# One reciprocal over 512 suffix products in place of the second scan of each attention chunk

## What is computed

```
state = zeros(B, H, D, D)
for t in range(S):
    state = alpha[:, :, t, :, None] * state + einsum('bhd,bhe->bhde', k[:, :, t], v[:, :, t])
    y[:, :, t] = einsum('bhd,bhde->bhe', q[:, :, t], state)
...
h = relu(xt @ w_tok1) @ w_tok2;  u = x + h.T
h2 = relu(u @ w_ch1) @ w_ch2;    x = u + h2
... then one expert (w1, w2) for each token, picked by a sticky gate
```

## Time and profile before

| | us |
|---|---|
| median of 3 runs | 518.74 (516.93 to 519.31) |
| profiled execution, its own time | 517.57 |
| its span, first to last instruction | 515.8 |
| PE busy in it | 455.6 (88%) |
| DVE busy in it | 273.6 (53%) |
| ACT, POOL busy in it | 175.1 (34%), 79.4 (15%) |

### The profile page before, as it was taken

How to read it: one execution, slowest core, us unless ns; L and a number is a source line. 1 busy time by engine, 2 the same in 40 slices (tenths; PEclk the granted TensorE clock), 3 DMA queues, 4 the chain that set the end, 5 groups by cost and what they waited for, 6 DMA issues and landing times.

```text
span 515.8 us, 8602 instructions
## 1 busy us (share of the span) xinstructions
PE 455.6 (88%) x2810; PEld 413.5 (80%) x2811; DVE 273.6 (53%) x519; ACT 175.1 (34%) x324; POOL 79.4 (15%) x108
## 2 busy tenths in 40 slices
PE   4889999999899999898999998309999999999992
PEld 3779999999799999898888997208888888887872
DVE  7649643654745633352666535742747557457320
ACT  1322153122231212341242321602755646557230
POOL 2060020021120002040222001350111110100100
PEclk9998999999999999898999999758999999999997
DMA  9995412307153007710402051216574563710110
GB/s 155 270 189 88 82 41 69 46 17 154 22 117 93 1 0 290 293 47 1 138 1 91 1 197 65 92 46 213 167 258 156 190 213 99 263 45 24 42 32 29
DMA packets 75200, 55.93 MB, mean 108 GB/s; under 512 B 52242, under 2 KB 70702, under 8 KB 75168
## 3 DMA queue, kind: packets, MB, share of 16 engines
q1 hardware_dynamic: 70992, 47.41, 34.0%
q0 software_dynamic: 1728, 4.73, 2.4%
q10 hardware_dynamic: 2448, 3.36, 2.4%
HBM read 48.99 MB, written 7.10 MB: 109 GB/s over the span
## 4 chain that ended last, share of the span: by engine, by line
PE 71%; DVE 10%; issue 9%; ACT 3%; DMA 2%; POOL 2%; ACTq 0%; DVEq 0%; POOLq 0%
PE bank L1044 20%; PE bank L1046 18%; PE bank L1045 17%; PE bank L1254 3%; PE bank L1112 3%; DMA sorted_rows<-vrow,idx_rows 2%; PE bank L1108 2%; PE bank L1144 2%; PE bank L1185 2%; PE bank L1097 1%; PE bank L1081 1%; ACT hc_hi L687 1%; DVE ms L837 1%; PE bank L1228 1%; DVE upto L818 1%
## 5 line engine op out<-in xcount | busy, mean ns | idle before, releaser
L882 DVE SCALAR_TENSOR_TENSOR hc_lo<-bank,hc_hi 128x384 fp32r<-128x384 f32 x48 | 26.4, 556 | 58.7 <-ACT hc_hi L687 58.5
L1044 PE MATMUL bank<-hc_hi,wc_hi 128*128 128x384 f32 x144 | 50.9, 354 | 4.0 <-DVE hc_lo L882 3.2
L1044 PE MATMUL bank<-ut_hi,wc_hi 128*128 128x384 f32 x144 | 49.7, 345 | 2.6 <-DVE vt L891 2.6
L687 ACT ACTIVATE hc_hi<-bank 128x384 fp32r<-128x384 f32 x48 | 23.2, 489 | 84.3 <-PE bank L1046 84.2
L1006 DVE TENSOR_TENSOR expert_parts<-raw_expert,expert_parts x72 | 45.4, 685 | 7.9 <-ACT expert_parts L742 7.9
L1046 PE MATMUL bank<-hc_hi,wc_lo 128*128 128x384 f32 x144 | 49.1, 341 | 0.0
L1045 PE MATMUL bank<-hc_lo,wc_hi 128*128 128x384 f32 x144 | 48.9, 340 | 0.0
L1046 PE MATMUL bank<-ut_hi,wc_lo 128*128 128x384 f32 x144 | 48.3, 335 | 0.0
L1045 PE MATMUL bank<-ut_lo,wc_hi 128*128 128x384 f32 x144 | 48.3, 335 | 0.0
L742 ACT CAST expert_parts<-raw_expert x72 | 39.2, 616 | 25.7 <-PE bank L1046 21.3
L1044 PE MATMUL bank<-expert_parts,hT_hi 128*128 (+1 forms) x120 | 44.7, 372 | 0.0
(11 more groups left out here) (181 smaller groups left out, 959.2 us busy)
## 6 DMA issues: line engine op xcount, KB each, us to landing
raw_expert<-in_moe_w SPq DMA_DIRECT2D x16, 1536.0 KB, 7.4
route_sb<-in_moe_w_ch SPq DMA_DIRECT2D x10, 576.0 KB, 5.2
raw_late<-in_moe_w_ch SPq DMA_DIRECT2D x6, 576.0 KB, 5.2
xg<-sorted_rows ACTq DMA_DIRECT2D x17, 193.0 KB, 2.4
ab<-in_alpha SPq DMA_DIRECT2D x12, 192.0 KB, 4.9
kb<-in_k SPq DMA_DIRECT2D x12, 192.0 KB, 4.8
qb<-in_q SPq DMA_DIRECT2D x12, 192.0 KB, 4.9
vb<-in_v SPq DMA_DIRECT2D x12, 192.0 KB, 3.3
```

Source lines behind the costliest of these rows:

```text
L687: a.activation(hc[0][:, s[3], :], src[:, 0:TW], ACT.Relu).then_inc(mix_hi, 1)
L882: ins = d.scalar_tensor_tensor(lo, src, 0.0, hi.bitcast(F32), ALU.max, ALU.subtract)
L1044: mm(dst, left[0], right[0], start=start, stop=False)
```

## The change

In each A(n) the small reciprocal and the forward scan go, and a reciprocal over the 512 suffix products writes `upto`. It stands behind `kn`. `later_ok` is raised by the backward scan rather than by the forward one, and DVE itself waits for it ahead of `kn`. `start_z` and its memset go; `upto` has 512 places rather than 517.

```
-        upto = take("upto", FLAT)
+        upto = take("upto", NP * P)
         ones_z = take("ones_z", FLAT)
-        start_z = take("start_z", FLAT)
...
-            put(d.memset(start_z, 0.0))
...
-                    link(d.tensor_tensor_scan(la[:, 0:FLAT - 1][:, ::-1], fl[:, 1:FLAT][:, ::-1],
-                                              ones_z[:, 1:FLAT][:, ::-1], 0.0, ALU.mult, ALU.add))
-                    if n:
-                        dve.wait_ge(qn_ok, n)
-                    ins = d.reciprocal(flat_zeros(start_z), flat_zeros(la))
-                    link(ins)
-                    d.tensor_tensor_scan(upto[:, 0:FLAT - 1], fl[:, 0:FLAT - 1], start_z[:, 0:FLAT - 1],
-                                         0.0, ALU.mult, ALU.add).then_inc(later_ok, 1)
+                    d.tensor_tensor_scan(la[:, 0:FLAT - 1][:, ::-1], fl[:, 1:FLAT][:, ::-1],
+                                         ones_z[:, 1:FLAT][:, ::-1], 0.0, ALU.mult, ALU.add).then_inc(later_ok, 1)
+                    dve.wait_ge(later_ok, n + 1)
                     dve.wait_ge(k_T, n + 1)
                     if n >= 2:
                         dve.wait_ge(sc_ok, n - 1)
                     d.tensor_tensor(pairs(kn[n % 2]), pairs(bank[1][:, :]), flat_steps(la), ALU.mult).then_inc(kn_ok, 1)
+                    if n:
+                        dve.wait_ge(qn_ok, n)
+                    link(d.reciprocal(pairs(upto), flat_steps(la)))
                     dve.wait_ge(q_T, n + 1)
-                    dve.wait_ge(later_ok, n + 1)
                     if n >= 3:
                         dve.wait_ge(y_ok, n - 2)
-                    d.tensor_tensor(pairs(qn[n % 3]), pairs(bank[2][:, :]), flat_steps(upto), ALU.mult).then_inc(qn_ok, 1)
+                    d.tensor_tensor(pairs(qn[n % 3]), pairs(bank[2][:, :]), pairs(upto), ALU.mult).then_inc(qn_ok, 1)
```

More of the change, by code:

```diff
@@ L324, in build @@
         N_CONST = 19
-        N_PADS = 12
+        N_PADS = 11
         in_a = [sem(f"in_a{i}") for i in range(2)]
```

## The result

| | before | after |
|---|---|---|
| median, us | 518.74 (516.93 to 519.31) | 534.51 (533.47 to 536.55) |
| ratio, with its 95% interval | | 1.0312 (1.0283 to 1.0341) |
| profiled execution, its own time | 517.57 | 536.55 |
| its span | 515.8 | 534.8 |
| mean granted clock of PE in it | 0.960 | 0.938 |

The change is slower by 15.8 us; 6.6 had been forecast, and the time lies just above the range. The two traces are 19.0 us apart, more than the medians: the trace of after is its slowest run, and that of before comes from an execution with a clock of 0.960, while 40 of the 56 runs of before that were made beside the experiments had 0.949 to 0.954 and 518.4 to 520.9 us.

The account below looks back on a forecast made before the run. DVE was taken to bound the rounds of chunks 4 to 6, PE 80 to 195 us. Early chunks 0.2, rounds 4.8 and chunk 9 1.6 summed to 6.6 us over 518.74, giving 525.3 us; range 520.5 to 534.

Parts of the forecast that it names:

- The closed loop of chunks 4 to 6: Rounds of DVE work, then POOL's `faded`, bound by DVE: each 1.60 us longer, 4.8 us for three.
- R: Duration of one DVE reciprocal over 512 elements, taken as 2.92 us; the edit costs R - 1.32 us a chunk.
- The three estimates of the slope: Reciprocal time per element from short instructions: 5 ns (two short reciprocals), 3.5 (against TENSOR_SCALAR), 7.5 (against COPY); 5.4 taken.
- The bounds of R: From 0.67 us, if the reciprocal streamed like `kn`, to 4.0 us, from the COPY comparison.
- chunks 0 to 2: DVE has room there; first masks end some 0.2 us after PE wants their banks, cost 0.2 us.
- the early chunks: Chunks at the start, before the closed loop: 0.2 us in the sum, 2.2 us at the range's high end.
- The clock fall as a side case: Rival: longer PE pauses bring one 1.2 GHz stretch where PE is the bound, 1.7 us more, 527.0; chance 0.12.
- The covers of chunks 7, 8, 10 and 11: `qn` ends later but before PE wants it for the scores, hidden by 0.3 to 0.5 us; cost 0.
- Chunk 3's state behind the weight split: State done at 37.0 us, POOL on its second weight split until 37.72; hidden with 0.7 us to spare, cost 0.
- The order: `kn` comes 0.78 us earlier, ahead of the reciprocal; buys nothing since PE needs `qn` for the scores.
- The memset: The removed memset (517 elements) runs while PE waits for its first DMA; cost 0.
- The rival "long reciprocal": 8.3 ns an element, 4.4 us per reciprocal; covers give way, 20.8 us more, 539.5 us; chance 0.15.

Follow-up runs that it names:

- e3: Changed kernel with the reciprocal over only 4 of the 512 products, the rest of `upto` kept at 1 (output differs): 533.09 us, ratio 1.026.
- e4: Changed kernel with idle repeats on PE at its pauses in chunks 1 to 6 and 9, DVE work the same: 528.07 us, ratio 1.0177.
- e5: Kernel before with both scans kept, only the small reciprocal and forward scan moved behind `kn`: 520.02 us, ratio 1.0006.
- e16: Kernel before with an extra 228-element reciprocal on DVE and idle repeats on PE, fewer than in a first try: 525.35 us, ratio 1.0136.
- e8: Kernel before with one more reciprocal on DVE, 228 elements into an unread tile, between `kn` and `qn`: 531.9 us, ratio 1.0255.
- e15: Changed kernel with POOL's two weight splits moved behind `faded` of chunk 5: 530.58 us, ratio 1.0245.

## Why the prediction was wrong

- **The closed loop of chunks 4 to 6: right.** It stayed a loop of DVE and POOL's `faded`; a round grew by R - 1.28 us, where R - 1.32 had been worked out (`kn` and `qn` are 0.01 to 0.02 us longer each; why is not shown, since `kn` kept its layout).
- **R: mis-sized.** 2.92 taken, 3.34 measured. The three estimates of the slope from instructions of 3 and 4 elements were 3.5, 5 and 7.5 ns; the slope is 6.25. The step between the two short rows was no measure of it: by the line through the long ones 3 and 4 elements would take 160 and 166 ns, and the rows have 176 and 181, while 4 elements took 171 in e3. What makes these few ns isn't shown. The bounds of R (0.67 to 4.0) held it. It makes 4 x 0.42 = 1.7 us, and about 1.1 more in chunks 0 to 2, where I had 0.2 and the trace 1.3. With R = 3.34 the sum of the prediction, the early chunks taken between its 0.2 and 2.2 us, would have been 1.0 + 6.1 + 2.0 + 0.6 = 9.7 us, 528.4 us in all, an estimate. That is what e4 measured with the clock kept up (528.07), and 6 us short of the changed kernel. So of the 9.2 us by which the forecast missed, some 3 are R and some 6 the clock.
- **The clock fall as a side case: the step that failed.** The sum put it at nothing and kept it as a rival, with a chance of 0.12, a single fall and a price of 1.7 us. The traced execution of after has three that cost: 2.1 us in chunk 1 to 3, 5.7 ahead of the token groups and 1.6 at chunk 9, 9.4 of the 19.0 us; without them the kernel takes 528.1 (e4), so by the medians they cost 6.4 of the 15.8 us. I had sized a fall by the one that the earlier trace rows show, 3.4 us long and hidden. The one at 66 us is 13 us long. And I had taken the pause of about 1 us between 80 and 195 us, which left the clock at 1.00, as evidence against, though the change makes pauses of 2.96 and 3.48 us. Such a pause was in my own sum: the masks late by 4.8 us, with PE waiting for them. And the trace of before does show dense work at the lower clock behind a long pause, in a part that the edit doesn't touch: PE waits 15.14 us for the first rows of the experts, and its matmuls then take 0.63 us until about 351.4, and 0.39 soon after.

```profile
346.56 0.87 PE L1228 MATMUL bank<-ident,xg 128*128 128x128 f32 x3 [15.14 <-DMA xg<-sorted_rows]
...
349.25 0.63 PE L1045 MATMUL bank<-expert_parts,xT_hi 128*128 128x512 f32 x1
...
351.71 0.39 PE L1045 MATMUL bank<-expert_parts,xT_hi 128*128 128x512 f32 x1
```

- **The covers of chunks 7, 8, 10 and 11: right.** The four together cost 0.4 us at R = 3.34, though the thin ones were passed: the weight loads of PE's scores wait for `qn` four times, 1.1 us in total and 0.3 at the longest.
- **Chunk 3's state behind the weight split: half right.** It hid behind the split, as said. But the split itself came 3.4 us late (37.66 instead of 34.29): it stands behind ACT's `wt_hi`, that behind the output of chunk 1, and that was on PE at the lower clock. In e4, with the clock up, the split starts at 35.52, so 2.1 of the 3.4 us are clock. I had followed DVE there and not PE.
- **The order: nothing,** as said (e5: 1.0006). The memset was not tested apart; the first scan of after starts at 5.79 us, that of before at 5.95.
- **The rival "long reciprocal"** gave 539.5 us, nearer to the 534.5 than my 525.3 and for a wrong reason: 8.3 ns an element. The Trainium skill (VectorE: DVE Perf Modes, "First, the fixed hardware budget") gives the repeat count of 8. The runs show 6.25 ns an element. With the 0.96 GHz of that page this makes an estimate of six cycles, not eight.

## What to carry to other kernels

In this kernel a delay on one engine was paid twice when it made a pause on TensorE ahead of dense work: once as the wait, and again as the stretch at the lower clock. By the medians the waits cost about 9 us here and the clock 6.4; with the reciprocal of 228 elements both were about 6.5 us (e16 over before, and e8 over e16). Before an edit that lengthens a side engine's chain, list the pauses of PE that it makes, not only the delays, and test such an edit with PE kept busy, to tell the two parts apart. Compare places in the traces too, and not only medians: what a fall costs differed from one execution to the next. A reciprocal on DVE is a slow instruction (6.25 ns an element here, against 2.4 of a scan, 1.23 us for 516): one over 4 elements and a scan over 512 beat one over 512.

## What the runs showed of the hardware

- The reciprocal on DVE takes 0.141 us and 6.25 ns an element (f32, from 192, 448 and 512 elements; 228 elements would be 1.566 and took 1.57).
- Ahead of the token groups PE paused for 3.48 us (after), and its clock was at 1.2 GHz for 13.7 us, 12.1 of them work without a further pause. At the same place it was 10.2 us with a pause of 2.84 (e8) and 3.4 with one of 2.14 (e15); at chunk 9 it was 3.4 us with a pause of 2.96 (after) and 6.8 with one of 2.97 (e15). So the length of the pause alone doesn't settle that of the stretch, and these runs don't show what does.
- A DVE scan with both inputs in SBUF and a POOL instruction hold each other up: 4.08 instead of 1.23 us, and 1.76 instead of 0.83.
